# Half of a weight-splitting step moved from VectorE to GpSimd in a fused recurrence and mixer kernel

## The chip, the cores and the metric

The kernel runs on one core of one Trainium2 chip. The metric is the device time of one execution in microseconds, on that core. A core has TensorE (PE in the profile), VectorE (DVE), ScalarE (ACT), GpSimd (POOL), and SyncE (SP), whose queue issues the loads here. Each engine works through its own queue in order; between engines there are semaphores.

## The reference

The inputs are four batches of 768 steps with 8 heads of 48 numbers. A recurrence with per-element decay runs first; two dense mixers follow on its output, viewed as 768 rows of 384.

```python
for t in range(S):                                   # recurrence, S = 768
    cur = einsum('bhd,bhe->bhde', u * kt, vt)
    y[:, :, t] = einsum('bhd,bhde->bhe', rt, state + cur)
    state = wt[..., None] * state + einsum('bhd,bhe->bhde', kt, vt)
x = y as (B, S, 384)
h = maximum(x.T @ w_tok1, 0) @ w_tok2                # w_tok1 768x256, w_tok2 256x768
u = x + h.T
x = u + maximum(u @ w_ch1, 0) @ w_ch2                # w_ch1 384x1536, w_ch2 1536x384
gate = sigmoid(5-tap causal convolution of x along S)
out = (gate * (x @ w_val)) @ w_out                   # both 384x384
```

All is float32.

## The kernel before

**Numbers in two parts.** The dense products use two-part numbers: a value is a rounded high part (fp32r, index `HI`) plus a low part, value minus high part (index `LO`). Each product is HIxHI + HIxLO + LOxHI. So every weight has to be split once at the start.

**The weight split.** The six weight matrices are cut into 20 chunks, numbered 0 to 19; sixteen are 128 partitions by 768 columns, and of val and outw the second chunks (17 and 19) are 128x384. For chunk n, SP loads it into one of two staging buffers: `gate` for even n, `xf` for odd n (both are real buffers of the last stage that are free until then). ScalarE copies it, rounded, to the HI part (`split_weight` at its line 453, which every ScalarE copy shows) and raises `w_hi`. Then VectorE subtracts, staging minus HI, into the LO part (line 580) and raises `w_lo[n % 2]`. SP's `load_weight(n)` waits on `w_lo[n % 2]`, so chunk n + 2 is loaded once chunk n is subtracted. Three readers wait on the counts of both semaphores: TensorE before the first product that needs a chunk, ScalarE before the first tap writes `gate`, and VectorE before the first write of `xf`. Below, w:n is the split of chunk n.

**The recurrence.** The 768 steps are worked in units of 256 steps (three in a batch, twelve in all, s = 0 to 11), in a doubling scheme: level products L1 to L32. For each level TensorE makes scores in PSUM; VectorE puts them under a mask into `at` (line 633, COPY_PREDICATED), multiplies `rk` by the decays (`carry`, line 574, 112x1024), and joins two decays to one (`join_decays`, line 574, `wp` or `w`, 512 down to 16 columns). GpSimd does two things: for F:s, `weigh` multiplies r and k by u (line 421, 112x1024), and for D:s, `states` walks the unit's four states, a decay product (line 438) and an addition (line 441) of 112x192 each. `states(s)` waits for ScalarE's copy of the state products, `ds_sb`. TensorE's outputs (A:s, B:s) wait for the states. Z:s takes the unit's output to `xs`, the dense part's input.

**The order.** `PROGRAM` is one list, written out by hand, that every engine walks in the same order and from which it takes what it has a part in. In the prologue and in the first trip the w:n stand between the level steps:

```python
    F:0 W:0 L2:0 L1:0 F:1 W:1 L4:0 w:0 L2:1 L8:0 L4:1 F:2 L1:1 w:1 W:2 L16:0 L8:1 L2:2 L1:2 w:2 w:3 L4:2 L16:1
    L32:0 L8:2 w:4 L32:1 T:0 L16:2 D:0 w:5 L32:2 T:1 w:6 D:1 A:0 T:2 B:0 A:1 Z:0 F:3 w:7 w:8 B:1 D:2 Z:1 P:0
    L1:3 A:2 w:9 W:3 L2:3 w:10 B:2 Z:2 P:1 L4:3 P:2 G1.0.0 G1.0.1
```

W:s is the first two decay joins and the carry of level 1. w:11 to w:19 stand in the first trip, in between the first batch's dense steps (U, C1, C2) and the fourth unit. Behind w:19 no weight is split; three batches of the recurrence and all of the dense work but the first pieces follow.

The dense steps: G1 and U are the token mixer, C1 and C2 the channel mixer (line 666 makes the low part of `hid`), X, tap, gate, V, M, S and O the second mixer. Every TensorE instruction shows line 755.

Of the kernel before, what the change touches and what calls it, by code (L numbers as in the profile page):

```python
# [5 lines left out]
F32 = mybir.dt.float32  # L6
F32R = mybir.dt.float32r
U8 = mybir.dt.uint8  # L8
ALU = mybir.AluOpType
# [16 lines left out]
HI, LO = 0, 1  # L26
# [106 lines left out]
def home(s):  # L133

    return {0: 1, 2: 2}.get(s, 0)


def tenant(s):

    if s < SUPERS:  # L140
        return 0
    return 2 if s == SUPERS else s
# [3 lines left out]
def landing(s):  # L146

    return {0: 2, 1: 0, 2: 3, 3: 1}.get(s, s % 2)


def landed_before(s):

    return {0: None, 1: None, 2: None, 3: None, 4: 1}.get(s, s - 2)


def landings(s):

    return 1 if s < 4 else s // 2 if s % 2 == 0 else (s - 1) // 2
# [29 lines left out]
def weight_chunks(tok1, tok2, ch1, ch2, val, outw):  # L188

    out = []  # L190
    for name, w, per in (("tok1", tok1, 3), ("tok2", tok2, 1), ("ch1", ch1, None), ("ch2", ch2, 2),
                         ("val", val, 2), ("out", outw, 2)):
        rows, cols = w.shape
        tiled = w.rearrange("(k p) n -> p k n", p=P)
        if per is None:
            for h in range(2):
                for k in range(rows // P):
                    out.append((name, k * cols + h * cols // 2, cols // 2,
                                tiled[:, k:k + 1, h * cols // 2:(h + 1) * cols // 2]))
        else:  # L200
            for k in range(0, rows // P, per):
                n = min(per, rows // P - k)
                out.append((name, k * cols, n * cols, tiled[:, k:k + n, :]))
    return out


def build(nc, rk, v, w, u, mask_d, ident_d, tok1_d, tok2_d, ch1_d, ch2_d, val_d, conv_d, outw_d, y_out):
    ctx = ExitStack()
    with ctx:
        def sb(name, shape, dt=F32):  # L210
            return ctx.enter_context(nc.sbuf_tensor(name, shape, dt))

        def sem(name):
            return ctx.enter_context(nc.semaphore(name))

        wt = {
            "tok1": sb("tok1", [P, 2, S // P * FT], F32R), "tok2": sb("tok2", [P, 2, FT // P * S], F32R),
            "ch1": sb("ch1", [P, 2, DT * FC], F32R), "ch2": sb("ch2", [P, 2, FC // P * DM], F32R),
        }
# [6 lines left out]
        stage = (gate[:, :], xf[:, :, :].rearrange("p d t -> p (d t)"))  # L226
# [48 lines left out]
        def decays(s, m):  # L275

            if m == 1:
                return w_sides[home(s)][0:RD, :]
            return wp_sides[home(s)][0:RD, W_AT[m]:W_AT[m] + PH * CH // m]
# [6 lines left out]
        w_hi, w_lo = sem("w_hi"), [sem("w_lo0"), sem("w_lo1")]  # L286
# [21 lines left out]
        chunks = weight_chunks(tok1_d, tok2_d, ch1_d, ch2_d, val_d, outw_d)  # L308
        NW = len(chunks)

        def need(engine, semaphore, count):

            if count > 0:
                engine.wait_ge(semaphore, count)

        def since(b, per_batch, count, times=1):

            return (b * per_batch + count) * times
# [33 lines left out]
        @block.sync  # L352
        def _(sp):
            def load_rk(s):

                b, i = divmod(s, SUPERS)
                at, before = landing(s), landed_before(s)
                if before is not None:
                    sp.wait_ge(y_done, 4 * (before + 1))
                    sp.wait_ge(ds_done, 4 * (before + 1))  # L360
                sp.dma_start(rk_sides[at][0:RD, :], rk[b, i]).then_inc(rk_in[at], 16)

            def load_w(s):

                b, i = divmod(s, SUPERS)
                need(sp, next_done[1], tenant(s))
                need(sp, decay_done[2], tenant(s))
                sp.dma_start(w_sides[home(s)][0:RD, :], w[b, i]).then_inc(decay_in[home(s)], 16)

            def load_v(s):  # L370

                b, i = divmod(s, SUPERS)
                need(sp, y_done, 4 * (s - 1))
                sp.dma_start(vs[:, s % 2, :, :].rearrange("p h d -> p (h d)"), v[b, i]).then_inc(v_in[s % 2], 16)

            def load_weight(n):
                need(sp, w_lo[n % 2], n // 2)
                name, c0, cols, src = chunks[n]
                sp.dma_start(stage[n % 2][:, 0:cols].rearrange("p (k n) -> p k n", k=src.shape[1]), src)\
                    .then_inc(w_in[n % 2], 16)  # L380

            sp.dma_start(ut[0:RD, :], u).then_inc(u_in, 16)
            load_rk(0)
            load_w(0)
            sp.dma_start(own_masks[:, :], mask_d).then_inc(mask_in, 16)
            sp.dma_start(ident[:, :], ident_d).then_inc(ident_in, 16)
            load_rk(1)
            load_w(1)
            load_weight(0)
            load_rk(2)  # L390
            load_w(2)
            load_v(0)
            load_weight(1)
            load_v(1)
            sp.dma_start(cw[:, :, :].rearrange("p d t -> p (d t)"), conv_d).then_inc(cw_in, 16)
            load_rk(3)
            for kind, n, name in PROGRAM:
                if kind == "weight" and n + 2 < NW:
                    load_weight(n + 2)
                elif kind == "att" and name == "W" and (n == 1 or 3 <= n < NS - 1):  # L400
                    load_w(max(n + 1, SUPERS))
                elif kind == "att" and name == "B":
                    if n == 1:
                        load_rk(4)
                    elif 3 <= n < NS - 2:
                        load_rk(n + 2)
                    if n + 2 < NS:
                        load_v(n + 2)
            for sc in range(2):
                sp.wait_ge(out_dma[sc], since(B, TILES, 0, times=16))  # L410

        @block.gpsimd
        def _(pool):
            def weigh(s):

                pool.wait_ge(rk_in[landing(s)], 16 * landings(s))
                need(pool, lev_done[1], 4 * tenant(s))
                plain, first = rk_sides[landing(s)][0:RD, 0:1], first_rk[home(s)][0:RD, 0:1]
                steps = [[PH * CH + 1, 2], [QS * CH, PAIRS], [2, SU // 2]]
                scale = bass.AP(ut.tensor, ut.offset, [[ut.ap[0][0], RD], [0, 2], [1, PAIRS], [0, SU // 2]])  # L420
                nc.gpsimd.tensor_tensor(bass.AP(first.tensor, first.offset, [list(first.ap[0])] + steps),
                                        bass.AP(plain.tensor, plain.offset, [list(plain.ap[0])] + steps),
                                        scale, ALU.mult).then_inc(weighed, 1)

            def states(s):

                first = QS * (s % SUPERS)
                need(pool, y_done, 4 * (s - 1))
                pool.wait_ge(decay_done[CH], s + 1)
                pool.wait_ge(ds_sb, s + 1)  # L430
                decay = decays(s, CH).rearrange("p (a q) -> p a q", q=QS)
                for q in range(chunks_of(s)):
                    now, new = st[0:RD, (first + q) % SLOTS], st[0:RD, (first + q + 1) % SLOTS]
                    if first + q == 0:
                        nc.gpsimd.tensor_copy(new, ds[0:RD, q]).then_inc(st_done, 1)
                    else:
                        pool.wait_ge(st_done, states_until(s, q))
                        nc.gpsimd.tensor_tensor(new, now, decay[:, :, q].unsqueeze(2).to_broadcast([RD, PAIRS, D]),  # L438
                                                ALU.mult).then_inc(st_decayed, 1)
                        pool.wait_ge(st_decayed, states_until(s, q) - s // SUPERS)  # L440
                        nc.gpsimd.tensor_tensor(new, new, ds[0:RD, q], ALU.add).then_inc(st_done, 1)

            pool.wait_ge(u_in, 16)
            for kind, n, name in PROGRAM:
                if kind == "att" and name == "F":
                    weigh(n)
                elif kind == "att" and name == "D":
                    states(n)
# [123 lines left out]
        def _(dve):  # L572
# [2 lines left out]

            def split_weight(n):

                name, c0, cols, _ = chunks[n]
                dve.wait_ge(w_hi, n + 1)
                nc.vector.tensor_tensor(wt[name][:, LO, c0:c0 + cols], stage[n % 2][:, 0:cols],  # L580
                                        wt[name][:, HI, c0:c0 + cols].bitcast(F32), ALU.subtract)\
                    .then_inc(w_lo[n % 2], 1)

            def join_decays(s, m):

# [468 lines left out]
```

## Time and profile before

| | us |
|---|---|
| median of three runs | 647.87 |
| lowest and highest | 647.32 to 650.0 |
| the profiled execution, whole | 647.32 |
| its span, first to last instruction | 645.3 |
| TensorE busy in the span | 606.6 |
| VectorE busy | 405.5 |
| ScalarE busy | 185.6 |
| GpSimd busy | 78.1 |

The span is what the trace covers; 2.0 us lie around it. TensorE is the fullest engine over the whole, but the share is a mean over an early part, in which the recurrence of the first three units runs with nothing else, and a later part, in which dense products fill TensorE. In a timeline row the first number is the start in us from the span's start, the second the duration in us, x the number of instructions merged, and in brackets stands how long the engine was idle before and who ended that. Consecutive instructions of an engine overlap a little in these rows.

### The profile page before, as it was taken

How to read it: one execution, taken by the hardware profiler on the slowest of the kernel's cores; microseconds unless marked ns; L12 is line 12 of the kernel's file. 1: busy time of each engine (PE TensorE's matmuls, PEld its weight loads, DVE VectorE, ACT ScalarE, POOL GpSimd, SP SyncE). 2: the span in 40 equal slices, each digit the busy share in tenths (PEclk: the TensorE clock that was granted, in tenths of full speed). 3: DMA queues.
4: the chain of work that ended last, by engine and by line, in shares of the span. 5: the costliest groups of instructions: out<-in, count | busy, mean ns of one | idle time of the engine just before them, and what ended most of it. 6: DMA issues, size and time to landing. Idle time of an engine off the chain costs nothing.

```text
span 645.3 us, 24065 instructions
## 1 busy us (share of the span) xinstructions
PE 606.6 (94%) x11150; PEld 584.9 (91%) x11150; DVE 405.5 (63%) x628; ACT 185.6 (29%) x323; POOL 78.1 (12%) x100
## 2 busy tenths in 40 slices
PE   3578888999999999999999999999999999999997
PEld 3577888999999999999999999999999989999997
DVE  6995387595677485586667475486666362452616
ACT  2135424134133133122233132123232132221312
POOL 2103501204003000304003000304002000000000
PEclk9999989999999999999999999999999999999999
DMA  9822534401203100301302200300000000000000
GB/s 241 244 76 68 153 120 134 127 4 49 90 3 97 42 6 25 112 3 32 107 4 70 68 1 29 112 4 3 26 3 2 26 25 1 2 1 25 1 25 25
DMA packets 13332, 35.27 MB, mean 55 GB/s; under 512 B 1584, under 2 KB 7984, under 8 KB 11888
## 3 DMA queue, kind: packets, MB, share of 16 engines
q1 hardware_dynamic: 9776, 29.01, 15.4%
q10 hardware_dynamic: 3456, 4.72, 2.1%
q8 instruction: 88, 1.44, 0.9%
q14 instruction: 12, 0.10, 0.0%
HBM read 29.01 MB, written 4.72 MB: 52 GB/s over the span
## 4 chain that ended last, share of the span: by engine, by line
PE 81%; DVE 10%; issue 4%; ACT 2%; DMA 2%; DVEq 1%; SPq 0%; ACTq 0%
PE ps L755 81%; DVE rk L574 2%; DMA w<-in_w_dram 1%; DVE gate L722 1%; DVE at L633 1%; DVE wp L574 1%; DVEq L697 1%; ACT x2s L453 1%; DVE us L681 1%; DMA xf<-in_moe_w_ch_dram 1%; DVE x2s L709 1%; DVE xf L698 1%; DVE rk_next L574 1%; DVE xf L702 1%; DVE ch L580 0%
## 5 line engine op out<-in xcount | busy, mean ns | idle before, releaser
L755 PE MATMUL ps<-us,ch 128*128 128x256 f32 x1296 | 166.7, 283 | 2.3 <-DVE us L681 1.4
L755 PE MATMUL ps<-hid,ch 128*128 128x256 f32 x1296 | 165.9, 283 | 0.0
L755 PEld LDWEIGHTS ps<-us,ch 128*128 128x128 f32 x1296 | 157.1, 188 | 5.3 <-DVE us L681 3.0
L755 PEld LDWEIGHTS ps<-hid,ch 128*128 128x128 f32 x1296 | 157.0, 188 | 1.8
L666 DVE SCALAR_TENSOR_TENSOR hid<-ps,hid 128x512 fp32r<-128x512 f32 x72 | 49.7, 691 | 125.6 <-ACT hid L523 125.5
L523 ACT ACTIVATE hid<-ps 128x512 fp32r<-128x512 f32 x72 | 43.0, 597 | 158.7 <-PE ps L755 158.7
L722 DVE SCALAR_TENSOR_TENSOR gate<-xf,cw,gate 128x256 f32<-128x256 f32 x144 | 72.4, 548 | 3.7 <-ACT gate L539 2.7
L755 PE MATMUL ps<-rk 48*64 48x32 f32 (+1 forms) x2240 | 48.0, 243 | 23.5 <-DVE rk L574 19.2
L755 PEld LDWEIGHTS ps<-rk 48*64 48x64 f32 (+1 forms) x2240 | 44.3, 162 | 28.0 <-issue 24.4
L574 DVE TENSOR_TENSOR rk<-rk,wp 112x1024 f32<-112x1024 f32 x35 | 44.5, 1274 | 11.5 <-PE ps L755 11.4
L438 POOL TENSOR_TENSOR st<-st,wp 112x192 f32<-112x192 f32 x40 | 24.7, 618 | 211.1 <-ACT ds L453 208.6
L755 PE MATMUL ps<-outw,x2s 128*128 128x384 f32 x216 | 40.3, 339 | 2.0 <-ACT x2s L453 1.8
L755 PE MATMUL ps<-x2s,val 128*128 128x256 f32 x324 | 41.4, 284 | 0.0
L755 PEld LDWEIGHTS ps<-x2s,val 128*128 128x128 f32 x324 | 39.9, 191 | 0.4
L574 DVE TENSOR_TENSOR rk_next<-rk_next,wp 112x1024 f32<-112x1024 f32 x25 | 30.5, 1221 | 14.9 <-PE ps L755 14.9
L755 PEld LDWEIGHTS ps<-outw,x2s 128*128 128x128 f32 x216 | 36.7, 188 | 3.1 <-DVE gate L574 2.2
L633 DVE COPY_PREDICATED at<-masks,ps 128x512 f32<-128x512 uint8 (+1 forms) x36 | 33.8, 938 | 4.9 <-PE ps L755 4.4
L755 PE MATMUL ps<-tok,h 128*128 128x256 f32 x216 | 31.4, 289 | 0.3 <-DVE h L666 0.2
L755 PEld LDWEIGHTS ps<-rk_next 48*64 48x64 f32 (+1 forms) x1600 | 23.9, 129 | 8.1 <-issue 6.2
L633 DVE COPY_PREDICATED at_next<-masks,ps 128x512 f32<-128x512 uint8 (+1 forms) x30 | 27.4, 914 | 6.2 <-PE ps L755 5.9
L755 PE MATMUL ps<-rk_next 48*64 48x32 f32 (+1 forms) x1600 | 26.7, 215 | 4.0 <-DVE rk_next L574 4.0
L755 PE MATMUL ps<-xs,tok 128*128 128x384 f32 x144 | 29.3, 364 | 0.0
(84 smaller groups left out, 615.0 us busy)
## 6 DMA issues: line engine op xcount, KB each, us to landing
rk<-in_rk_dram SPq DMA_DIRECT2D x7, 896.0 KB, 8.5
w<-in_w_dram SPq DMA_DIRECT2D x12, 448.0 KB, 3.7
vs<-in_v_dram SPq DMA_DIRECT2D x12, 384.0 KB, 6.9
out_dram<-gate ACTq DMA_DIRECT2D x24, 192.0 KB, 1.9
rk_next<-in_rk_dram SPq DMA_DIRECT2D x5, 896.0 KB, 7.1
gate<-in_moe_w_ch_dram SPq DMA_DIRECT2D x6, 384.0 KB, 3.9
xf<-in_moe_w_ch_dram SPq DMA_DIRECT2D x6, 384.0 KB, 3.8
gate<-in_moe_w_tok_dram SPq DMA_DIRECT2D x2, 384.0 KB, 9.0
```

Of the source, the lines that this page charges most:

```text
L438: nc.gpsimd.tensor_tensor(new, now, decay[:, :, q].unsqueeze(2).to_broadcast([RD, PAIRS, D]), ALU.mult).then_inc(st_decayed, 1)
L453: return nc.scalar.activation(out, in_, ACT.Copy)
L523: nc.scalar.activation(hid[:, HI, g % 2, :], ps[:, RING + use % 2, :], ACT.Relu)\
L574: return nc.vector.tensor_tensor(out, a, b_, ALU.mult)
L633: nc.vector.copy_predicated(out, may.unsqueeze(1).to_broadcast(list(out.shape)), src)\
L666: return nc.vector.scalar_tensor_tensor(out, bank, 0.0, hi.bitcast(F32), ALU.max, ALU.subtract)
L681: nc.vector.tensor_tensor(us[:, LO, dts, :], bank, us[:, HI, dts, :].bitcast(F32), ALU.subtract).then_inc(ring_free[use % 2], 1)
L697: dve.drain()
L698: nc.vector.tensor_tensor(xf[:, :, HALO:], us[:, HI, :, :].bitcast(F32), us[:, LO, :, :].bitcast(F32), ALU.add)
L702: nc.vector.tensor_tensor(xf[:, 0:2, HALO:], ps[:, ACC, :].rearrange("p (d t) -> p d t", d=2), xf[:, 0:2, HALO:], ALU.add).then_inc(x2_don ...
L722: nc.vector.scalar_tensor_tensor(gate3[:, dt, :], xf[:, dt, k:k + TT], cw[:, dt, k:k + 1], gate3[:, dt, :], ALU.mult, ALU.add).then_inc(ta ...
L755: return nc.tensor.matmul(out, lhsT, rhs, start=start, stop=stop, skip_group_check=True, **kw)
```

## The change

The subtractions of the odd chunks, those staged in `xf`, go from VectorE's queue to GpSimd's: w:1, w:3 and so on to w:19, eight of 128x768 and two of 128x384. Operands, result and semaphores are the same (`w_hi` waited for, `w_lo[1]` raised). VectorE keeps the even chunks. On GpSimd the subtraction stands where w:n stands in `PROGRAM`, in between `weigh` and `states`. SP, ScalarE and TensorE have the same rows as before.

```diff
         @block.gpsimd
         def _(pool):
+            def split_weight(n):
+                if n % 2 == 1:
+                    name, c0, cols, _ = chunks[n]
+                    pool.wait_ge(w_hi, n + 1)
+                    nc.gpsimd.tensor_tensor(wt[name][:, LO, c0:c0 + cols], stage[1][:, 0:cols],
+                                            wt[name][:, HI, c0:c0 + cols].bitcast(F32), ALU.subtract)\
+                        .then_inc(w_lo[1], 1)
+
...
             for kind, n, name in PROGRAM:
-                if kind == "att" and name == "F":
+                if kind == "weight":
+                    split_weight(n)
+                elif kind == "att" and name == "F":
                     weigh(n)
...
             def split_weight(n):
 
-                name, c0, cols, _ = chunks[n]
-                dve.wait_ge(w_hi, n + 1)
-                nc.vector.tensor_tensor(wt[name][:, LO, c0:c0 + cols], stage[n % 2][:, 0:cols],
-                                        wt[name][:, HI, c0:c0 + cols].bitcast(F32), ALU.subtract)\
-                    .then_inc(w_lo[n % 2], 1)
+                if n % 2 == 0:
+                    name, c0, cols, _ = chunks[n]
+                    dve.wait_ge(w_hi, n + 1)
+                    nc.vector.tensor_tensor(wt[name][:, LO, c0:c0 + cols], stage[0][:, 0:cols],
+                                            wt[name][:, HI, c0:c0 + cols].bitcast(F32), ALU.subtract)\
+                        .then_inc(w_lo[0], 1)
```

VectorE at w:2 and w:3, in the prologue, before. Each row is an instruction with its tiles, shape and the semaphores it waits for:

```order
L633 COPY_PREDICATED at<-masks,ps 128x1024 [waits into_done3,lev_done1]
L580 TENSOR_TENSOR tok<-gate,tok 128x768 [waits w_hi]
L580 TENSOR_TENSOR tok<-xf,tok 128x768 [waits w_hi]
L574 TENSOR_TENSOR rk<-rk,wp 112x2x128x4 [waits decay_done4,lev_done4]
L574 TENSOR_TENSOR wp<-wp 112x64 [waits decay_done8]
```

The same place of the change (lines are 10 or 11 higher there):

```order
L644 COPY_PREDICATED at<-masks,ps 128x1024 [waits into_done3,lev_done1]
L591 TENSOR_TENSOR tok<-gate,tok 128x768 [waits w_hi]
L584 TENSOR_TENSOR rk<-rk,wp 112x2x128x4 [waits decay_done4,lev_done4]
L584 TENSOR_TENSOR wp<-wp 112x64 [waits decay_done8]
L644 COPY_PREDICATED at<-masks,ps 128x128x4 [waits into_done3,lev_done4]
```

The subtraction from `xf` is gone and the carry of L4:2 follows w:2 at once.

VectorE at w:9, before, where the fourth unit begins:

```order
L633 COPY_PREDICATED at_next<-masks,ps 128x1024 [waits zero_done,lev_done1]
L580 TENSOR_TENSOR ch<-xf,ch 128x768 [waits w_hi]
L574 TENSOR_TENSOR wp<-w 112x512 [waits decay_in0]
L574 TENSOR_TENSOR rk_next<-rk_next,w 112x2x512 [waits plain_done,rk_in1]
L574 TENSOR_TENSOR wp<-wp 112x256 [waits decay_done2]
```

and in the change:

```order
L644 COPY_PREDICATED at_next<-masks,ps 128x1024 [waits zero_done,lev_done1]
L584 TENSOR_TENSOR wp<-w 112x512 [waits decay_in0]
L584 TENSOR_TENSOR rk_next<-rk_next,w 112x2x512 [waits plain_done,rk_in1]
L584 TENSOR_TENSOR wp<-wp 112x256 [waits decay_done2]
L584 TENSOR_TENSOR rk_next<-rk_next,wp 112x2x256x2 [waits weighed,decay_done2,lev_done2]
```

W:3 follows the masked copy of L1:3 directly.

GpSimd from the third `weigh` (F:2) to the first state product of the second unit. Before, with the states' repeats left out:

```order
L421 TENSOR_TENSOR fk<-rk,ut 112x2x512 [waits rk_in3]
L435 COPY st<-ds 112x192 [waits ds_sb,decay_done64]
...
L438 TENSOR_TENSOR st<-st,wp 112x192 [waits st_done]
L441 TENSOR_TENSOR st<-st,ds 112x192 [waits st_decayed]
L438 TENSOR_TENSOR st<-st,wp 112x192 [waits st_done,ds_sb,decay_done64]
```

and in the change:

```order
L429 TENSOR_TENSOR fk<-rk,ut 112x2x512 [waits rk_in3]
L418 TENSOR_TENSOR tok<-xf,tok 128x768 [waits w_hi] x2
L443 COPY st<-ds 112x192 [waits ds_sb,decay_done64]
...
L446 TENSOR_TENSOR st<-st,wp 112x192 [waits st_done]
L449 TENSOR_TENSOR st<-st,ds 112x192 [waits st_decayed]
L418 TENSOR_TENSOR ch<-xf,ch 128x768 [waits w_hi]
L446 TENSOR_TENSOR st<-st,wp 112x192 [waits st_done,ds_sb,decay_done64]
```

w:1 and w:3 stand before the first unit's states, w:5 between the first unit's and the second's.

## Rows read from the trace of the kernel before

**Rows 1.** The page's chain of work that ended last, by engine

```profile
PE 81%; DVE 10%; issue 4%; ACT 2%; DMA 2%; DVEq 1%; SPq 0%; ACTq 0%
```

**Rows 2.** Busy time of each engine by stretch, one stretch of the prologue

```profile
core 0: us, PE busy (x) PEld busy (x) DVE busy (x) ACT busy (x) POOL busy (x), PEclk, DMA share, GB/s
...
27.00:53.00 26.00, 21.68 (x819) 20.81 (x819) 25.39 (x34) 8.70 (x16) 0.00 (x0) 1.00 0.26 76
```

**Rows 3.** The tile xf until 250 us: duration min/median/max, first and last start

```profile
L580 DVE TENSOR_TENSOR ch<-xf,ch x6: 943/959/1126, 56.8 to 107.2; 128x768 fp32r<-128x768 f32 x6
...
L580 DVE TENSOR_TENSOR tok<-xf,tok x2: 931/940/948, 33.3 to 44.1; 128x768 fp32r<-128x768 f32 x2
```

**Rows 4.** GpSimd's lines 421 and 441, columns as in group 3

```profile
L421 POOL TENSOR_TENSOR fk<-rk_next,ut x5: 1898/1905/2108, 68.4 to 447.8; 112x1024 f32<-112x1024 f32 x5
...
L441 POOL TENSOR_TENSOR st<-st,ds x40: 587/630/1460, 57.2 to 488.2; 112x192 f32<-112x192 f32 x40
```

**Rows 5.** Timeline, two places: start us, us, instruction, idle before and its releaser

```profile
13.40 2.66 POOL L421 TENSOR_TENSOR fk<-rk,ut 112x1024 f32<-112x1024 f32 x1 [4.20 <-DMA rk<-in_rk_dram]
...
14.23 1.99 DVE L574 TENSOR_TENSOR wp<-wp 112x128 f32<-112x128 f32 x1
...
115.80 1.91 POOL L421 TENSOR_TENSOR fk<-rk,ut 112x1024 f32<-112x1024 f32 x1
...
115.98 0.69 DVE L666 SCALAR_TENSOR_TENSOR hid<-ps,hid 128x512 fp32r<-128x512 f32 x1 [0.60 <-ACT hid L523]
116.59 1.54 DVE L580 TENSOR_TENSOR val<-xf,val 128x384 fp32r<-128x384 f32 x1
```

**Rows 6.** Timeline around w:1 and w:3

```profile
24.65 0.84 ACT L453 ACTIVATE tok<-xf 128x768 fp32r<-128x768 f32 x1 [2.97 <-DMA xf<-in_moe_w_tok_dram]
...
25.25 1.21 DVE L574 TENSOR_TENSOR rk<-rk,wp 112x1024 f32<-112x1024 f32 x1
26.39 0.28 DVE L574 TENSOR_TENSOR wp<-wp 112x128 f32<-112x128 f32 x1
...
30.02 1.23 DVE L574 TENSOR_TENSOR rk<-rk,wp 112x1024 f32<-112x1024 f32 x1 [0.40 <-PE ps L755]
...
37.37 0.16 DVE L574 TENSOR_TENSOR wp<-wp 112x16 f32<-112x16 f32 x1
...
46.96 2.94 PE L755 MATMUL ps<-rk 48*64 48x32 f32 x128 [1.66 <-DVE at L633]
```

**Rows 7.** Timeline around w:5 and w:6

```profile
61.52 1.03 DVE L580 TENSOR_TENSOR ch<-gate,ch 128x768 fp32r<-128x768 f32 x1 [2.08 <-ACT ch L453]
...
63.44 0.51 POOL L438 TENSOR_TENSOR st<-st,wp 112x192 f32<-112x192 f32 x1 [1.71 <-ACT ds L453]
...
66.56 0.59 POOL L441 TENSOR_TENSOR st<-st,ds 112x192 f32<-112x192 f32 x1
...
67.29 1.16 PE L755 MATMUL ps<-vs,at 64*64 64x48 f32 x32
```

**Rows 8.** Timeline around w:9

```profile
77.17 0.60 POOL L441 TENSOR_TENSOR st<-st,ds 112x192 f32<-112x192 f32 x1
...
79.67 0.94 DVE L580 TENSOR_TENSOR ch<-xf,ch 128x768 fp32r<-128x768 f32 x1
...
82.50 1.14 PE L755 MATMUL ps<-rk_next 48*64 48x32 f32 x64 [3.26 <-DVE rk_next L574]
```

**Rows 9.** Timeline around w:11 and w:13

```profile
92.20 0.84 ACT L453 ACTIVATE ch<-xf 128x768 fp32r<-128x768 f32 x1
...
93.68 1.22 DVE L574 TENSOR_TENSOR rk_next<-rk_next,wp 112x1024 f32<-112x1024 f32 x1
...
95.52 0.94 DVE L580 TENSOR_TENSOR ch<-xf,ch 128x768 fp32r<-128x768 f32 x1
...
101.54 0.96 DVE L580 TENSOR_TENSOR ch<-xf,ch 128x768 fp32r<-128x768 f32 x1 [0.55 <-ACT ch L453]
...
104.38 1.15 PE L755 MATMUL ps<-ident,rk_next 48*64 48x48 f32 x64 [0.92 <-DVE rk_next L574]
```

**Rows 10.** Busy time by stretch, columns as in group 2, behind w:9

```profile
80.00:84.00 4.00, 1.50 (x101) 1.53 (x104) 2.94 (x5) 0.00 (x0) 0.00 (x0) 1.00 0.76 219
84.00:86.00 2.00, 2.00 (x43) 1.91 (x35) 2.00 (x3) 0.81 (x1) 0.00 (x0) 0.51 0.53 176
```

## The prediction, made before the changed kernel was run

> **What bounds the kernel now.** I read the page first: the chain of work that ended last is TensorE for 81% and VectorE for 10% [rows 1]. So an edit on VectorE counts only where TensorE stands still for it. Then the busy times by stretch: in 27 to 53 us VectorE works 25.39 of 26.00 us while TensorE works 21.68 [rows 2]. The prologue is bound by VectorE, and from about 105 us on TensorE is dense. All ten moved subtractions lie before 134 us; the batches behind that are untouched, so what the change does is a shift of the point at which the dense part begins.
>
> **What is moved.** Ten odd chunks, w:1 to w:19. VectorE sheds two of 940 ns (w:1, w:3) and six of 959 ns (w:5 to w:15) [rows 3], and two narrow ones (w:17, w:19). Since neighbours on VectorE overlap a little (in [rows 6] the operation that starts at 25.25 with 1.21 us is followed at 26.39), one wide subtraction is worth 0.87 us of its queue.
>
> **What one costs on GpSimd.** No row shows GpSimd on 768 columns. The nearest: 1024 columns take 1.905 us in `weigh` (its second input repeats four values), and the 192-column state add, with two full inputs, 0.587 us at its fastest [rows 4]. The straight line through both gives 0.587 + 576 x (1.905 - 0.587) / 832 = 1.50 us; four state adds give 2.35 us. I take 1.7, nearer the low end since a fixed part is paid once, above it since the weighed row reads one full input only. Ends kept: 1.5 and 2.35.
>
> The Trainium skill, "GPSIMD Engine Reference", section 3.1, gives 4497 ns for an fp32 tensor_tensor add of 2048 columns and calls VectorE about twice as fast; an estimate from it for 768 columns is 1.69 us, by which the sum below would be the same.
>
> **Does the work really leave VectorE?** This decides the case. At 13.40 a `weigh` took 2.66 us instead of 1.90, with a VectorE product of two SBUF operands running as it began; and the 128-column decay product that VectorE issued at 14.23 took 1.99 us, ending when GpSimd ended. At 115.80 GpSimd ran 1.91 us undisturbed and the 384-column subtraction at 116.59 took 1.54 us, again ending behind it; yet the `hid` operation at 115.98, which reads PSUM and one SBUF operand, took its usual 0.69 [rows 5]. So while GpSimd is in a two-operand operation, a VectorE operation with two SBUF operands stands still for the rest of it, and the reverse. Operations that read PSUM go on. Where VectorE's queue is full of decay products and carries, a move swaps 0.87 us of work for up to 1.7 us of standstill.
>
> The Trainium skill, "SBUF — State Buffer", section "SBUF: two separate sides", speaks of an exclusive lock: the first to start has the shared port pair for its whole instruction. By that rule the masked copies, whose data come from PSUM, run on. No row here has one beside a GpSimd operation; if they were stopped too, w:9 below would lose its gain.
>
> **The sum, place by place.** *w:1.* ScalarE's half ends at 24.65 + 0.84 = 25.49. VectorE's carry holds until 26.39; GpSimd is waiting and goes next, 26.4 to 28.1, and the decay product of 26.39 waits, with the whole queue behind it: +1.7. Before the carry at 30.02 VectorE idled 0.40 for TensorE, which absorbs that much; then 0.87 is shed: +0.43. *w:3.* Its load goes out earlier, since SP waits on w:1. GpSimd is ready near 37, waits for a carry, and stops the product of 37.37: +1.7 - 0.87 = +0.83, with nothing idle until TensorE, which had stood still 1.66 us for VectorE's mask, starts at 46.96 [rows 6]. Together +1.26. I charge it whole.
>
> *w:5.* It stands on GpSimd between the first unit's states and the second's. GpSimd was free 1.71 us before 63.44, just the length of w:5. But VectorE's w:6 comes at 61.52 and contends. If it goes first, w:5 runs from 62.4 to 64.1 and the second unit's states begin 0.65 us late; if w:5 is first, w:6 runs until about 63.8 and the states' first product waits 0.35 for it. TensorE's next outputs at 67.29 follow the third state of that unit, which ended at 66.56 + 0.59 = 67.15 [rows 7]: nearly no slack. +0.4. On SP the load behind w:5 moves to about 63 us and that behind w:6 waits with it; ScalarE wants those chunks only after F:3, which stands three stages on, so I charge nothing and leave it to the range.
>
> *w:7* falls between F:3's `weigh` and the third unit's states, where both queues have room: nothing. *w:9* is the place where the change gains. GpSimd ends the states at 77.17 + 0.60 and does w:9 until 79.5; VectorE only has a masked copy then, and comes to the decay products 0.86 us earlier, at 79.67 where w:9 stood. TensorE stood 3.26 us for them, until 82.50 [rows 8]: -0.86.
>
> *w:11.* ScalarE ends at 92.20 + 0.84 = 93.04; VectorE is in another two-operand operation until its carry; GpSimd goes 93.65 to 95.35, just ahead of the carry at 93.68: +1.7, and w:11 at 95.52 is shed: +0.83. VectorE then has no idle time but 0.55 us before w:13 (101.54). *w:13* stops one more decay product; the idle time and the shed 0.87 pay for most: +0.3. TensorE waited 0.92 us on VectorE at 104.38, so both reach it [rows 9]: +1.13. *w:15* and *w:17* find VectorE waiting: nothing. *w:19* stops a decay product while TensorE has some slack: 0 to 0.4, I take 0.2.
>
> Sum: 1.26 + 0.40 - 0.86 + 1.13 + 0.20 = +2.1 us. The profiled execution took 647.32, its span 645.3 and 2.0 around it, so the forecast is 649.4 us. The median of the three runs shown is 647.87, 0.55 above it; against that the change is +1.5 us, 0.24%.
>
> **One term I cannot place.** In 80 to 84 us TensorE worked 1.50 of 4.00, and in 84 to 86 its granted clock was 0.51, which is the 1.2 GHz level, with 2.00 of 2.00 busy [rows 10]. If w:9's shorter gap keeps it at 2.4 GHz, about half of those two us and a bit of the next come back: -1.2. If the longer gaps near 100 to 105 bring such a drop, +1.2. I take 0 and keep both ends.
>
> **Rivals.** *A, exclusion at 1.7 us, as above:* 649.4, by the duration's low end and the clock's gift 647.32 + 2.1 - 5 x 0.2 - 1.2 = 647.2, by mild excess 651.1. Chance 0.60.
>
> *B, slower: GpSimd is the long link.* Place: w:5 ahead of the second unit's states, then the same excess at w:1, w:3, w:11, w:13. It decides once a subtraction takes over about 2.0 us, because then even unhindered w:5 ends after 63.44. At 2.35 us: w:1 and w:3 2 x 1.48 - 0.40 = 2.56; w:5 behind 61.73 until 64.08, w:6 behind it, states 1.0 late; w:9 ends at 80.1, gain only 0.4; w:11 and w:13 about 1.48 + 0.95 = 2.4; w:19 0.4. Sum +6.0: 653.3 us. For it: the state add's rate. Against it: the `weigh` row. Chance 0.20.
>
> *C, the delays are taken up.* TensorE's own queue has waits that VectorE's rows don't explain, and the wait of 1.66 us at 46.96 has a mask as its releaser, so the order of things there may shift. If the +1.26 of the early part vanishes, 2.1 - 1.3 = +0.8 is left, 648.1 us; with w:11's 0.83 gone too it is 647.3. I put it at 647.7. Chance 0.12.
>
> *D, the move works as it reads: GpSimd hides it all.* This needs the exclusion to be absent. Then w:1 and w:3 give 1.66 (no more than TensorE's wait at 46.96), w:9, w:11 and w:13 0.87 each: -4.3, 643.0 us. Against it stand all of [rows 5]. Chance 0.08.
>
> **How the numbers follow.** This measurement can tell about 0.5%, 3.2 us, from no change: the bounds are 644.6 and 651.1. *Same*: C 0.12, 0.52 of A, 0.03 of a weak D: 0.67. *Slower*: B 0.20, and 0.07 of A (gaps and clock together): 0.27. *Faster*: 0.06, D with a little of A's clock gift. The range leaves out D and the upper half of B: 646.6 to 652.6.
>
> **What would show it.** After the change: GpSimd rows of 128x768 near 1.7 us, more where VectorE held first; 112x128 and 112x16 decay products on VectorE near 26.4 and 38 us stretched to 1.5 us and over; TensorE's run at 46.96 later by 1.3; its outputs at 67.29 later by 1.7; the run at 82.50 by 0.8 only; that at 104.38 by 1.9 or so, and the dense part in one piece behind it. Stretched rows absent would mean D; subtractions of over 2 us and a late unit-1 state mean B; a shift that shrinks where no gain was due means C. A granted clock of 1.00 in 84 to 86 would take 1.2 us off.

## The result, and the profile after

| | before | after |
|---|---|---|
| median of ten runs, us | 648.48 | 652.39 |
| lowest and highest | 647.32 to 650.53 | 650.83 to 656.93 |
| ratio, 95% interval | 1 | 1.0073 (1.0051 to 1.0093) |
| profiled execution, span | 647.32, 645.3 | 653.66, 651.9 |
| mean granted clock of it | 0.997 | 0.992 |

The change costs 0.73%, some 4.7 us. The ratio rests on more executions than the table's two times ten, the change has 27 in it; the two medians by themselves are 3.9 us apart. The forecast was 649.4, 0.24% over the median then known. The direction holds and the time lies inside the range, but the effect is three times the forecast, so the forecast was wrong in size. More runs also raised the median of before: the profile from which I worked is its fastest execution of the ten.

The page of the kernel after, busy time by engine and the chain that ended last (against [rows 1]). GpSimd has 19 us more and VectorE 5 us more, not less, though VectorE has ten operations fewer: standstill counts as busy time. In a second profile of each kernel VectorE has 407.7 us before and 405.0 after, so the 5 us are partly scatter; of the some 9 us of shed operations it saves 2.7 at the most.

```profile
PE 605.5 (93%) x11150; PEld 583.3 (89%) x11150; DVE 410.1 (63%) x618; ACT 185.2 (28%) x323; POOL 97.2 (15%) x110
...
PE 80%; DVE 11%; issue 4%; ACT 2%; DMA 1%; DVEq 1%; POOL 1%; SPq 0%; ACTq 0%; POOLq 0%
```

VectorE and GpSimd in the kernel after, at w:1, w:3, w:9, w:11 and w:13 (start, duration):

```profile
25.92 2.18 POOL L418 TENSOR_TENSOR tok<-xf,tok 128x768 fp32r<-128x768 f32 x1 [2.17 <-ACT tok L463]
26.36 1.89 DVE L584 TENSOR_TENSOR wp<-wp 112x128 f32<-112x128 f32 x1
...
38.11 2.44 POOL L418 TENSOR_TENSOR tok<-xf,tok 128x768 fp32r<-128x768 f32 x1 [10.01 <-ACT tok L463]
38.78 1.81 DVE L584 TENSOR_TENSOR wp<-wp 112x32 f32<-112x32 f32 x1
...
77.75 1.30 DVE L644 COPY_PREDICATED at_next<-masks,ps 128x1024 f32<-128x1024 uint8 x1 [1.08 <-PE ps L766]
78.89 1.82 POOL L418 TENSOR_TENSOR ch<-xf,ch 128x768 fp32r<-128x768 f32 x1
78.94 2.32 DVE L584 TENSOR_TENSOR wp<-w 112x512 f32<-112x512 f32 x1
...
95.48 2.34 POOL L418 TENSOR_TENSOR ch<-xf,ch 128x768 fp32r<-128x768 f32 x1 [14.77 <-ACT ch L463]
96.04 2.85 DVE L584 TENSOR_TENSOR rk_next<-rk_next,wp 112x1024 f32<-112x1024 f32 x1
...
101.81 2.14 POOL L418 TENSOR_TENSOR ch<-xf,ch 128x768 fp32r<-128x768 f32 x1 [3.99 <-ACT ch L463]
102.18 2.85 DVE L584 TENSOR_TENSOR rk_next<-rk_next,wp 112x1024 f32<-112x1024 f32 x1
```

A subtraction on GpSimd takes 1.82 us undisturbed. The 128-column decay product, 0.28 us in [rows 6], takes 1.89; carries go from 1.22 [rows 9] to 2.85. That is the standstill of [rows 5].

TensorE in the kernel after, the rows that answer to [rows 6] to [rows 9]:

```profile
48.32 2.94 PE L766 MATMUL ps<-rk 48*64 48x32 f32 x128 [1.19 <-DVE at L644]
...
68.98 0.68 PE L766 MATMUL ps<-vs,at 64*64 64x48 f32 x32 [1.29 <-POOL st L449]
...
73.84 0.39 PE L766 MATMUL ps<-vs,rk 64*48 64x48 f32 x13 [0.97 <-issue]
74.16 2.35 PE L766 MATMUL ps<-xs,tok 128*128 128x384 f32 x12
...
82.54 1.60 PE L766 MATMUL ps<-rk_next 48*64 48x32 f32 x64 [2.31 <-DVE rk_next L584]
...
86.26 1.09 PE L766 MATMUL ps<-st,rk 48*64 48x48 f32 x27 [1.04 <-issue]
87.28 3.52 PE L766 MATMUL ps<-xs,tok 128*128 128x384 f32 x12
...
95.41 1.67 PE L766 MATMUL ps<-tok,h 128*128 128x256 f32 x12 [0.20 <-DVE h L677]
...
105.18 0.75 PE L766 MATMUL ps<-rk_next 48*32 48x32 f32 x64 [2.37 <-DVE rk_next L584]
105.85 3.38 PE L766 MATMUL ps<-us,ch 128*128 128x256 f32 x18
109.16 1.64 PE L766 MATMUL ps<-ident,rk_next 48*64 48x48 f32 x64
```

The shift against before is 1.36 us at the run of 128, 1.69 at A:1 (68.98 against 67.29), 0.04 at L2:3 (82.54 against 82.50), and 4.78 at T:3 (109.16 against 104.38); 1.3, 1.7, 0.8 and 1.9 were forecast. A part of what lies between the last two is a stall of 1.04 us without a releaser and the two carries of 2.85 us. Another is in the busy times by stretch: the granted clock, last column but two, is at its lower level, 1.2 GHz, far longer than in [rows 10], and again near 105 us.

```profile
80.00:84.00 4.00, 1.69 (x85) 1.59 (x79) 2.73 (x3) 0.00 (x0) 0.71 (x1) 0.87 0.99 255
84.00:86.00 2.00, 1.22 (x44) 1.06 (x38) 1.76 (x3) 0.00 (x0) 0.00 (x0) 0.50 1.00 221
86.00:90.00 4.00, 3.74 (x36) 3.65 (x37) 2.61 (x3) 0.81 (x1) 0.00 (x0) 0.52 0.49 142
...
105.00:110.00 5.00, 4.82 (x114) 4.59 (x118) 4.04 (x8) 1.44 (x2) 0.00 (x0) 0.69 0.32 85
```

### The profile page after: what moved, and what is told of

Same layout as the page of the kernel before. It is cut to its first block, busy times and chain, and to the rows that moved or that the text cites. A ratio compares the mean times of both kernels' runs of the same rounds, so it can differ in the third digit from the quotient of the medians.

```text
span 651.9 us, 24065 instructions
## 1 busy us (share of the span) xinstructions
PE 605.5 (93%) x11150; PEld 583.3 (89%) x11150; DVE 410.1 (63%) x618; ACT 185.2 (28%) x323; POOL 97.2 (15%) x110
## 3 DMA queue, kind: packets, MB, share of 16 engines
q8 instruction: 88, 1.44, 0.9%
## 4 chain that ended last, share of the span: by engine, by line
PE 80%; DVE 11%; issue 4%; ACT 2%; DMA 1%; DVEq 1%; POOL 1%; SPq 0%; ACTq 0%; POOLq 0%
PE ps L766 80%; DVE rk L584 2%; DVE wp L584 2%; DVE at L644 1%; DMA w<-in_w_dram 1%; DVE gate L733 1%; DVE rk_next L584 1%; DVEq L708 1%; DVE us L692 1%; ACT x2s L463 1%; DVE x2s L720 1%; DVE xf L709 1%; DVE xf L713 1%; DVE gate L584 0%; DVE x_sum L673 0%
## 5 line engine op out<-in xcount | busy, mean ns | idle before, releaser
L584 DVE TENSOR_TENSOR rk<-rk,wp 112x1024 f32<-112x1024 f32 x35 | 42.9, 1229 | 14.1 <-PE ps L766 14.1
L584 DVE TENSOR_TENSOR rk_next<-rk_next,wp 112x1024 f32<-112x1024 f32 x25 | 33.8, 1351 | 16.9 <-PE ps L766 16.9
L766 PEld LDWEIGHTS ps<-outw,x2s 128*128 128x128 f32 x216 | 36.7, 188 | 3.1 <-DVE gate L584 2.2
L449 POOL TENSOR_TENSOR st<-st,ds 112x192 f32<-112x192 f32 x40 | 28.3, 707 | 3.1
```

The costliest lines, as they stand in the source:

```text
L584: return nc.vector.tensor_tensor(out, a, b_, ALU.mult)
L766: return nc.tensor.matmul(out, lhsT, rhs, start=start, stop=stop, skip_group_check=True, **kw)
```

## The experiments

**The change in three parts.** In each only the named chunks go to GpSimd:

```diff
-                if n % 2 == 1:
+                if n in MOVED:      # (1, 3), then (5, 7, 9), then (11, 13, 15, 17, 19)
```

> Only w:1 and w:3 are subtracted on GpSimd, all else as before. Theory 1 (standstill by place: while GpSimd is in its subtraction, VectorE's operations on two SBUF operands wait): about +1.4 us over the kernel before, made of 1.8 us of standstill twice less 0.87 us of shed work twice, less 0.4 of idle time; visible as TensorE's run of 128 near 47 us starting at about 48.3. Theory 2 (the loss is GpSimd's own queue, states that come late behind a subtraction): 0, since no state stands behind w:1 or w:3. Theory 3 (all of the loss comes from TensorE's clock drop near 84 us growing longer): under 0.5 us here unless the granted clock of 80 to 90 us changes.

> Only w:5, w:7 and w:9 on GpSimd. Theory 1: w:5 and w:6 together make the second unit's states about 0.4 late, w:9 gains at most 0.9 if it ends before the mask of L1:3 does: between -0.5 and +0.5 us. Theory 2: this part alone carries the loss of the whole change, +3 to +4 us. Theory 3 (clock): +1 to +2 us, with a granted clock near 0.5 over more of 82 to 90 us than the two to three us of before.

> Only w:11, w:13, w:15, w:17 and w:19 on GpSimd. Theory 1: +2.0 to +2.5 us, from w:11 and w:13 that stop the carries of L8:3 and L16:3, each stretched to 2.8 us; w:15 and w:17 nothing; plus up to 0.9 us if the longer wait ahead of L32:3 lowers TensorE's clock for a while near 105 us. Theory 2 (late states): 0. Theory 3 (clock only, at 84 us): 0.

Measured, twelve runs each against 35 of before: w:1 and w:3 1.0031 (1.0004 to 1.0059), 2.0 us; w:5 to w:9 1.0007 (0.9983 to 1.003); w:11 to w:19 1.0045 (1.0021 to 1.0069), 2.9 us. The three add up to 0.83%, the whole change has 0.73%. The parts with standstill carry the loss; the middle part, in which the states of the second unit and w:9 lie, carries nearly none, so late states, which were to cost 3 to 4 us there, are out as the main cause. The clock alone is out too: it was to cost nothing in the last part. The prices of theory 1 fit, 1.4 us and 2.0 to 2.5 us each within the interval; these intervals are some 3 us wide, so they say where the loss lies and not how large each part is.

**No SBUF read on GpSimd.**

```diff
-                    nc.gpsimd.tensor_tensor(wt[name][:, LO, c0:c0 + cols], stage[1][:, 0:cols], ...)
+                    for part in range(4):
+                        a0, wide = c0 + part * cols // 4, cols // 4
+                        ins = nc.gpsimd.memset(wt[name][:, LO, a0:a0 + wide].bitcast(F32), 0.0)
...
```

> All odd chunks as in the change, but GpSimd writes zeros into the low part in four pieces (memset) where it subtracted, so it reads no SBUF; the low parts of the odd chunks are left out of the result. Waits and semaphores as in the change. Theory 1: VectorE's two-operand operations are not stretched, the shed work comes back as time: 2 to 4 us faster than the kernel before, 643 to 646 us. If the standstill came from any GpSimd operation, or if the loss were the order of GpSimd's queue or the hand-over through semaphores, it stays near the change, +2 to +4 us over before.

Measured: 1.0009 (0.9988 to 1.003), 650.22 us; the hoped gain isn't there, but neither is the loss. The four memsets take 0.85 us together, so this kernel differs from the change in length as well as in reading, and the low parts of the odd chunks are left out of its result. Its timelines, GpSimd, VectorE and TensorE:

```profile
27.61 0.85 POOL L420 MEMSET tok<- 128x192 f32 x4 [3.54 <-ACT tok L464]
...
27.97 1.25 DVE L585 TENSOR_TENSOR rk<-rk,wp 112x1024 f32<-112x1024 f32 x1
...
45.41 2.40 PE L767 MATMUL ps<-rk 48*64 48x32 f32 x88 [0.28 <-DVE at L645]
...
49.48 0.76 PE L767 MATMUL ps<-rk 48*32 48x32 f32 x40 [1.66 <-issue]
...
86.64 1.09 PE L767 MATMUL ps<-st,rk 48*64 48x48 f32 x27 [2.88 <-issue]
```

The memsets lie beside VectorE's operations and stretch none of them: the carry of 27.97, with the memsets of 27.61 beside it, takes 1.25 us, as before (27.67 there), and the 32-column product of 37.51 takes 0.19 us beside those of 37.36 (0.18 before). TensorE starts its run at 45.41, 1.55 us before [rows 6]: that is rival D's first term, 1.66, nearly whole. Then it stands 1.66 us at 49.48 and 2.88 at 86.64 with no engine as releaser ("issue"), and by the first token product (95.84, against 93.04 and 94.24 in two profiles of before) the gain is gone. Over the twelve runs the shed VectorE work was worth nothing that can be told, even with no operation standing still. That the stalls take it up is read from one profile and isn't shown.

**Before once more, unedited.**

> The kernel before once more, for a second profile. Every kernel with moved subtractions shows TensorE standing without a releaser behind the fifth matmul of B:2's state part (1.04 us in the change, 3.19, 1.78 and 2.88 in three of the four part kernels), the first profile of before shows none. If that stall belongs to the moved work, it is absent here too and the span is about 645 us. If it is the supply of TensorE's instructions, queued behind the loads near 73 to 84 us, it can appear here as well, at the same instruction, with a span of 646 to 649 us. Time ratio 1.000 within 0.3%.

Measured: 0.9976 (0.9948 to 1.0004), span 647.2. TensorE in this second profile of before:

```profile
78.86 1.14 PE L755 MATMUL ps<-rk_next 48*64 48x32 f32 x64 [1.55 <-DVE rk_next L574]
...
83.95 1.09 PE L755 MATMUL ps<-st,rk 48*64 48x48 f32 x27 [2.90 <-issue]
84.97 4.21 PE L755 MATMUL ps<-xs,tok 128*128 128x384 f32 x12
...
80.00:84.00 4.00, 1.10 (x41) 0.94 (x36) 3.41 (x4) 0.00 (x0) 0.00 (x0) 0.50 0.92 237
```

L2:3 comes 3.6 us earlier than in the first profile, and P:1 (84.97) at the same time as in it (84.91 there). The stall behind the fifth state matmul of B:2 is not the change's. It stands at the same instruction in before (2.90 us), in the change (1.04), in the first two part kernels (3.19 and 1.78) and in the memset kernel (2.88). It is absent in the first profile of before, and also in the second profile of the change and in the third part kernel: it comes in some executions and not in others, whatever the kernel. From the one profile in which I worked I couldn't see that it exists.

**Idle matmuls against the low clock.** Ahead of L2:3 (12 in before, 10 in the change) and ahead of L32:3 (9, in the change only), with results that the next stage overwrites:

```diff
                     if before:
                         pe.wait_ge(*emptied(*before))
+                    for n in range({(3, 'L2'): 12}.get((s, name), 0)):
+                        mm(ps[:, bank, 0:DM], wcols("tok1", HI, 0), xs[:, HI, 0, :], n == 0, n == 11)
```

> The kernel before with 12 idle matmuls of 128x384 in the wait ahead of L2:3 (near 80 us); their result is overwritten. If the clock drop near 84 us follows from TensorE's idle time there, the granted clock stays at 1.00 over 84 to 90 us and the kernel gains 1 to 2 us. If stalls without releaser come at fixed places of the instruction stream, the one in B:2 moves 12 matmuls to the front, from behind the fifth matmul of the state part into the part with the masked scores. If neither, the time is that of before.

> The change with 10 idle matmuls ahead of L2:3 and 9 ahead of L32:3. Theory that the lower clock (80 to 90 and 105 to 110 us) is a part of the loss: granted clock near 1.00 there, 2 to 3 us faster than the change, so +1 to +2 us over before. Theory that standstill and stalls alone make the loss: the time of the change, +4 to +5 us over before.

Measured: on before 0.9958 (0.9938 to 0.9979), 647.33 us, which beats both kernels; on the change 1.0052 (1.0021 to 1.0084). In before with idle matmuls, the clock and the stall:

```profile
84.00:86.00 2.00, 0.75 (x40) 0.69 (x39) 2.00 (x3) 0.00 (x0) 0.00 (x0) 1.00 0.58 201
...
85.25 0.27 PE L755 MATMUL ps<-vs,at 64*64 64x48 f32 x4 [1.25 <-issue]
85.98 2.37 PE L755 MATMUL ps<-xs,tok 128*128 128x384 f32 x12
```

The clock stays up, P:1 takes 2.37 us instead of 3.52, and the stall has moved: 28 records into the 32 of the masked scores, where it was 5 behind them. That is nine records for the twelve that were expected. Elsewhere in the change such stalls lie 128 matmul records apart: three records into A:1's state part, then 35 into D:2, which is 29 + 64 + 35 = 128. Both fit places that are fixed in TensorE's instruction stream; the count of nine fits only roughly. The page of the kernel after, its table of DMA queues (packets, MB, share), shows how the instructions come:

```profile
q8 instruction: 88, 1.44, 0.9%
```

1.44 MB in 88 packets is 16 KB each. The Trainium skill, "Runtime: NRT & Kernel Launch", section "Instruction fetch mechanics", says that a queue refills each engine's instruction memory in blocks of 16 KiB, 256 instructions, and calls the cost of crossing a block mostly hidden. A matmul and its weight load are two instructions, so 128 records are such a block; the trace agrees on the spacing, and if these stalls are such crossings, it doesn't on "mostly hidden": 2.90 us in b2 while the DMA engines are 0.92 busy.

On the change the gain is the smaller, 0.2% with intervals that overlap, though the clock was 1.00 in its profile; over its twelve runs the mean granted clock ranged from 0.990 to 1.000. The expectation of 2 to 3 us isn't met. The two kernels with idle matmuls can be compared as well: 652.07 against 647.33 us, 4.7 us apart, with intervals that don't meet. With idle matmuls in both, the change costs as much as without.

**Fewer bytes beside the stall.**

```diff
-                    if n == 1:
+                    if n == 2:
                         load_rk(4)
```

> The kernel before with the load of the fifth unit's rk (896 KB) behind B:2 instead of B:1 on SP, some 14 us later, still before F:1 of the first trip needs it. Theory that TensorE's instructions queue behind the loads of 73 to 84 us: no stall in B:2, TensorE's P:1 at or before the time of before, gain 0.5 to 2 us in the median. If the loads have nothing to do with it: no change.

Measured: 1.0006 (0.9983 to 1.003). Its profile has no stall in B:2 and P:1 begins early, but D:2 waits for its own load:

```profile
70.92 0.61 PE L755 MATMUL ps<-vs,rk 64*48 64x48 f32 x35 [0.51 <-DMA vs<-in_v_dram]
...
83.19 3.29 PE L755 MATMUL ps<-xs,tok 128*128 128x384 f32 x12
```

The runs show no gain, and the stall is absent in profiles of unedited kernels too, so that the loads of 73 to 84 us hold up the instructions isn't shown.

**w:11 and w:13 apart, and the change once more.**

```diff
+MOVED = (11,)        # and (13,) in the second
```

> Only w:11 on GpSimd. Read by the distance between the first token product (tok,h) and TensorE's L32:3, which was 7.37 us in both profiles of the kernel before and 9.77 us in the change. Theory: the carry of L8:3 waits 1.63 us for GpSimd, 0.87 is shed, so the distance is 7.37 + 0.77 = 8.1 us. If w:11 made the whole loss it would be 9.8.

> Only w:13 on GpSimd. With w:11 on VectorE the load of chunk 13 starts late, GpSimd subtracts only after the carry of L16:3 has run: distance from the first token product to L32:3 unchanged at 7.4 us, and T:3 at most 0.4 us later behind L32:3 than the 3.97 us of before. If w:13 costs its standstill wherever it stands, the distance is 9.0 us. Then the 2.40 us of the change would be the plain sum of two moves; by the theory it is more than that sum, since only together does w:13 fall ahead of the carry.

> The change once more for a second profile. The standstill terms repeat to 0.1 us: L32:3 9.77 us behind the first token product, the run of 128 matmuls some 37.3 us behind TensorE's first matmul. What varies is the stall behind the fifth state matmul of B:2 and the time at the lower clock, mean granted clock 0.982 to 0.995.

One execution each: 651.22 us, 651.30 us, and 651.12 us for the change; a single time can't rank them. w:11 alone (GpSimd, TensorE), then w:13 alone (GpSimd, VectorE, TensorE):

```profile
94.93 2.33 POOL L419 TENSOR_TENSOR ch<-xf,ch 128x768 fp32r<-128x768 f32 x1 [17.27 <-ACT ch L464]
...
94.86 1.69 PE L767 MATMUL ps<-tok,h 128*128 128x256 f32 x12 [0.20 <-DVE h L678]
...
103.00 0.75 PE L767 MATMUL ps<-rk_next 48*32 48x32 f32 x64 [0.72 <-DVE rk_next L585]
106.29 1.15 PE L767 MATMUL ps<-ident,rk_next 48*64 48x48 f32 x64 [0.24 <-DVE rk_next L585]
```

```profile
103.16 1.84 POOL L419 TENSOR_TENSOR ch<-xf,ch 128x768 fp32r<-128x768 f32 x1 [24.38 <-ACT ch L464]
...
104.20 1.88 DVE L585 TENSOR_TENSOR rk_next<-rk_next,wp 112x1024 f32<-112x1024 f32 x1
...
94.11 1.67 PE L767 MATMUL ps<-tok,h 128*128 128x256 f32 x12 [0.20 <-DVE h L678]
...
101.48 0.75 PE L767 MATMUL ps<-rk_next 48*32 48x32 f32 x64 [0.71 <-DVE rk_next L585]
106.23 1.15 PE L767 MATMUL ps<-ident,rk_next 48*64 48x48 f32 x64 [1.68 <-DVE rk_next L585]
```

Distance from the first token product to L32:3: w:11 alone 8.14 (expected 8.1), w:13 alone 7.37 (expected 7.4), both 9.77 in the change and, in its second profile, 9.77 again (93.82 to 103.59). The run of 128 came 36.70 us behind TensorE's first matmul in that second profile, not the 37.3 expected, so this distance repeats to 0.6 us and not to 0.1. The 2.40 us at L32:3 is more than the sum of the moves, 0.77: only when w:11 has been done early does chunk 13 arrive before the carry of L16:3 and stop it, and the work shed by w:13 lies behind that carry, too late to pay. At T:3 some of it comes back. From the first token product to T:3: before 11.34 and 11.55 (11.00 to 12.03 in four more kernels that leave both chunks alone), w:11 alone 11.43, w:13 alone 12.12 (over the 0.4 I had allowed), the change 12.78 in its second profile and 13.75 in its first, where C1.0.1 ran 3.38 us at the lower clock.

**A version that beats both, carried on.** Idle matmuls on before, and w:12 moved behind L16:3:

```diff
-    L8:0 w:11 U.0.0 w:12 L16:0 w:13 C1.0.0
+    L8:0 w:11 U.0.0 L16:0 w:12 w:13 C1.0.0
```

> The kernel before with 12 idle matmuls ahead of L2:3 and w:12 moved behind L16:3 in the order of all engines. Idle matmuls alone gave a ratio of 0.9958. Moving w:12 takes one subtraction of 0.87 us out of the way of the carry of L16:3, for which TensorE waits 0.72 us: first token product to L32:3 6.65 instead of 7.37 us, ratio 0.993 to 0.996. If TensorE is held by something else there, the ratio stays at 0.996.

Measured: 0.9966 (0.9945 to 0.9987), 647.46 us, against 0.9958 with the idle matmuls alone. In its profile L32:3 comes 6.59 us behind the first token product, near the 6.65 expected, so the wait there did go; but the two kernels can't be told apart in time, and the order adds nothing that these runs resolve.

## Why the prediction was wrong in size

Distances between TensorE's starts, in us, from the timelines. "Others unchanged" are kernels in which the stretch isn't touched; idle matmuls ahead of L2:3 count as touching the second stretch, and so does the later load of d1:

| stretch | before, both profiles | others unchanged | change, both profiles |
|---|---|---|---|
| first matmul to the run of 128 | 35.92, 35.29 | 35.37 to 35.90 | 37.30, 36.70 |
| run of 128 to first token product | 46.08, 48.07 | 46.98 to 49.64 | 47.09, 46.09 |
| first token product to T:3 | 11.34, 11.55 | 11.00 to 12.03 | 13.75, 12.78 |

*What GpSimd takes.* 1.82 us against 1.7 taken, inside 1.5 to 2.35. The estimate from the Trainium skill, "GPSIMD Engine Reference", section 3.1, was 1.69 and as near.

*Standstill.* Right: the stretched rows are there, and the memsets stretch none. The second stretched product is the one of 32 columns at 38.78 and not the one of 16 that I had named. The masked copies, for which no row of before had a case, aren't stopped: in the second profile of the change, shown under w:9, one takes 1.31 us beside a subtraction, as in before.

*w:1 and w:3, +1.26.* Measured 1.36 on the two profiles as read; with both profiles of each, 37.0 - 35.6 = 1.4; with the part kernel and the idle-matmul kernel that also move them (36.66, 36.25) and the nine profiles that don't, 36.7 - 35.6 = 1.1. Right.

*w:5, +0.4.* TensorE waited 1.29 us for the states at A:1, as the step said; but in the second profile of before it waited 1.59 there without w:5. No cost of w:5 can be told from that.

*w:9, -0.86: the step that failed.* I had GpSimd free before VectorE came to the decay products, and counted the credit as sure. In the result's profile GpSimd had ended the third unit's states only at 78.93 and VectorE its mask near 78.94, so w:9 began at 78.89 and the product stood until it ended, 2.32 us. From the start of the mask to TensorE's L2:3 it is 4.03 us in before and 4.79 there: +0.76 in place of -0.86. The second profile of the change shows the other outcome. First before (P:0 on TensorE, the mask), then that second profile (P:0, w:9, the mask, the product, L2:3):

```profile
73.02 4.21 PE L755 MATMUL ps<-xs,tok 128*128 128x384 f32 x12
...
78.47 1.31 DVE L633 COPY_PREDICATED at_next<-masks,ps 128x1024 f32<-128x1024 uint8 x1 [2.97 <-PE ps L755]
```

```profile
74.59 4.11 PE L766 MATMUL ps<-xs,tok 128*128 128x384 f32 x12
...
79.29 1.82 POOL L418 TENSOR_TENSOR ch<-xf,ch 128x768 fp32r<-128x768 f32 x1
...
79.93 1.31 DVE L644 COPY_PREDICATED at_next<-masks,ps 128x1024 f32<-128x1024 uint8 x1 [2.85 <-PE ps L766]
81.14 0.67 DVE L584 TENSOR_TENSOR wp<-w 112x512 f32<-112x512 f32 x1
...
83.09 1.14 PE L766 MATMUL ps<-rk_next 48*64 48x32 f32 x64 [2.39 <-DVE rk_next L584]
```

Here the product takes its usual 0.67 us, and from the mask to L2:3 it is 3.16 us: the credit of 0.87 is there, as in the middle part kernel (3.18) and in the change with idle matmuls (3.09). By the rows, what decides is TensorE's P:0 ahead of the mask; no run forces it either way. It took 4.21 us in the profile I worked from and 4.04 to 4.21 in the three with the credit; it took 2.35 in the profile without it, and there the mask came early, while GpSimd still had the states to do. In six of the nine profiles that leave w:9 on VectorE P:0 takes 2.35 to 2.89 us, so the execution I read was the rarer kind, and nothing in the sum said that the credit hung on it. (4.21 us for these twelve matmuls is what they take at a granted clock of 0.50, at 84.97 in the second profile of before. In the first one the clock's column reads 1.00 at 73.02 all the same, so it can't be relied on there.) The shift of 0.04 us at L2:3 in the result's profile is luck, shifts that cancel: P:0 begins 1.14 us later than in before, takes 1.86 less, and the way from the mask is 0.76 longer. How much of the credit, won or lost, reaches the dense part stays open: from P:0 to P:1 it is 13.12 and 10.72 us in the change and 11.89 and 13.72 in before.

*w:11 and w:13, +1.13.* Measured at T:3 about 1.3 (12.78 against 11.34 and 11.55). The size is near; the way isn't: I had w:13 behind the carry and it came ahead of it.

*The clock, taken as 0 with both ends kept.* In the result's profile the unfavourable end, +1.2, was what happened, near 82 to 90 us and again near 105; in the second profile of the change the drop near 105 is absent. The mean granted clock of the executions was 0.995 in the median for 35 runs of before and 0.992 for 27 of the change. 0.003 of 652 us at half clock is 3.9 us more at 1.2 GHz, and work bound by TensorE loses half of such time, so 2.0 us at the most. The executions put it lower. Among those of one kernel (184 of seven kernels, none with idle matmuls) the time grows by 0.20 us for each 0.001 that the mean granted clock falls, with a standard error of 0.04, which makes 0.6 us of 0.003. The change's ten executions with 0.994 and more have a median of 653.3 us, the 56 such of before, from other sets, 649.4: at an equal clock the difference is still there, as it is with idle matmuls in both kernels. So taking the clock as 0 was short by about 0.6 us, not by 2; what the column leaves out, as at 73.02 above, isn't in this.

*The base.* I added 2.1 us to 647.32, the lowest of the ten executions of before in the result. The kernel's medians over the sets were 648.48 to 650.32. Against the median then known this made the forecast +1.5 us instead of +2.1.

*w:15 to w:19, +0.2.* From T:3 to the next unit's outputs near 157 us the change takes 52.66 and 53.15 us, before 52.13 and 51.98, but kernels that leave these chunks alone take 52.07 to 53.01. No cost can be told.

So the rows show 1.1 to 1.4 us at w:1 and w:3 and 1.3 at w:11 and w:13, where I had 2.4 for both together: these prices were right. Measured are 4.7, with an interval of 3.3 to 6.0, where the sum had 2.1. Of the 2.6 us that it lacked, 0.9 is the credit of w:9 where it doesn't come and 1.6 where it turns into a loss, and about 0.6 is the clock. An execution like the result's profile then makes 1.1 to 1.4, 0.8, 1.3 and 0.6, which is 3.8 to 4.1 us and inside the interval; one in which w:9 gains makes 2.1 to 2.4 and isn't. This is a sum over places read in a few profiles: how many executions are of each kind, what the stalls take up, and where the rest lies stays open. Rival B had the right side and size, 653.3, but not its mechanism: GpSimd took 1.8 us, under its point of decision. Rival C's absorption didn't happen to the losses at w:1, w:3 and w:11; whether the stalls without a releaser absorb gains is open. D fell.

## What to carry to other kernels

Moving a two-operand SBUF operation from VectorE to GpSimd can only help where VectorE's next operations read PSUM or nothing; elsewhere count the whole GpSimd duration as VectorE's, 1.8 us here against 0.87 shed. A credit that rests on the order in which two queues arrive needs the question what sets that order: here it was how long one TensorE product took, 2.35 or 4.2 us, and that differed between executions of one kernel. Before pricing a change of half a percent, take a second profile of the same kernel: stalls without a releaser and the clock moved single places here by 3 us and more.

## What the runs showed of the hardware that I had not expected

TensorE stands still with no engine to blame, for 0.2 to 3.2 us (3.19 with w:1 and w:3 moved), at places of which several lie about 128 matmul records apart; the same place stalls in one execution of a kernel and not in the next (2.90 us and none in before, 1.04 and none in the change). TensorE's idle time ahead of L2:3, 1.55 to 3.26 us, is followed in every profile without idle matmuls by 3 to 14 us at a granted clock near 0.5, and 12 idle matmuls in it were worth 0.42% of a 650 us kernel. A VectorE operation on two SBUF operands waits for the whole of a GpSimd subtraction (0.28 to 1.89 us, 1.22 to 2.85), a masked copy of PSUM doesn't (1.31 beside a subtraction and without one), and memsets on GpSimd don't stop a carry (1.25 beside them and without).
